# Attention scores in two halves of TensorE's rows, softmax kept in PSUM, one PSUM bank for the input products, and another order of the attention steps

## What is computed

```python
scores = scale * np.matmul(q, k.transpose(0, 1, 3, 2))
keep = is_global | is_local          # first 8 keys, or the 96 keys up to the query
bias = -slopes[:, None, None] * dist[None, :, :]
scores = np.where(keep, scores + bias[None], -1000000000.0)
a = np.exp(scores - np.max(scores, axis=-1, keepdims=True))
a = a / (np.sum(a, axis=-1, keepdims=True) + 1e-09)
x = np.matmul(a, v)                  # then as tokens x 512
h = x @ w_in;  g = np.maximum(h, 0.0) + alpha * np.minimum(h, 0.0);  x = g @ w_out
h = x @ w_in2; g = P(h) / (Q(h) + 1e-06);                            out = g @ w_out2
```

## Time and profile before

| | us |
|---|---|
| Median of 3 runs (647.35 to 648.41) | 648.3 |
| The profiled execution's own time | 649.04 |
| Its span in the profile | 647.2 |
| PE busy | 627.8 |
| DVE, ACT, POOL busy | 460.3, 312.1, 286.8 |

### The profile page before, as it was taken

How to read it: one execution, slowest core, us unless ns; L and a number is a source line. 1 busy time by engine, 2 the same in 40 slices (tenths; PEclk the granted TensorE clock), 3 DMA queues, 4 the chain that set the end, 5 groups by cost and what they waited for, 6 DMA issues and landing times.

```text
span 647.2 us, 9416 instructions
## 1 busy us (share of the span) xinstructions
PE 627.8 (97%) x3048; PEld 503.8 (78%) x3048; DVE 460.3 (71%) x753; ACT 312.1 (48%) x664; POOL 286.8 (44%) x231
## 2 busy tenths in 40 slices
PE   6988999999999999999999999999999999999995
PEld 4666777777877777778888888888888888888884
DVE  6868776665476666646555559988869988599884
ACT  6853333333233333322111167866668766687662
POOL 4777650000000000001444468887757777587772
PEclk9999999999999999999999999999999999999999
DMA  5873321111011111010232210000010000100001
GB/s 161 234 224 102 94 63 37 50 30 30 0 28 42 43 28 39 0 46 20 98 97 99 97 66 0 2 1 1 1 65 0 0 0 0 65 2 0 1 1 69
DMA packets 38933, 31.28 MB, mean 48 GB/s; under 512 B 9008, under 2 KB 33264, under 8 KB 38896
## 3 DMA queue, kind: packets, MB, share of 16 engines
q1 hardware_dynamic: 38896, 30.83, 15.7%
HBM read 27.67 MB, written 3.15 MB: 48 GB/s over the span
## 4 chain that ended last, share of the span: by engine, by line
PE 90%; DVE 3%; issue 2%; DMA 2%; SPq 1%; ACT 1%; POOL 1%; DVEq 0%; POOLq 0%; ACTq 0%
PE ps_h L565 29%; PE ps_y L598 20%; PE ps_y L600 19%; PE ps_o L565 5%; PE ps_s L565 5%; PE ps_s L517 3%; PE ps_o L538 3%; PE ps_o L527 2%; DMA kT<-in_k 2%; PE ps_y L484 1%; SPq L375 1%; DVE g L1010 1%; PE ps_o L508 1%; PE ps_h L496 0%; PE ps_y L482 0%
## 5 line engine op out<-in xcount | busy, mean ns | idle before, releaser
L1227 POOL TENSOR_TENSOR win_lo<-stage,win_hi 128x1024 fp32r<-128x1024 f32 x8 | 19.2, 2405 | 229.9 <-DVE win_hi L1002 229.9
L565 PE MATMUL ps_h<-xy_hi,win_hi 128*128 (+1 forms) x288 | 118.5, 412 | 0.7 <-DVE xy_lo L944 0.7
L565 PE MATMUL ps_h<-xy_lo,win_hi 128*128 (+1 forms) x288 | 112.6, 391 | 0.0
L565 PE MATMUL ps_h<-xy_hi,win_lo 128*128 (+1 forms) x288 | 112.4, 390 | 0.0
L732 ACT ACTIVATE g_hi<-g 128x512 fp32r<-128x512 f32 x48 | 30.3, 631 | 134.7 <-PE ps_y L598 124.1
L1026 DVE RECIPROCAL ps_h<-denom 128x512 f32<-128x512 f32 x24 | 80.6, 3360 | 17.2 <-POOL denom L1234 16.6
L1234 POOL TENSOR_TENSOR denom<-denom,q_abs 128x512 f32<-128x512 f32 x48 | 62.6, 1305 | 62.5 <-ACT denom L752 62.5
L1019 DVE TENSOR_TENSOR g_lo<-g,g_hi 128x512 fp32r<-128x512 f32 x48 | 35.0, 729 | 64.6 <-ACT g_hi L732 64.6
L598 PE MATMUL ps_y<-g_hi,wout_hi 128*128 128x512 f32 x192 | 80.9, 422 | 0.0
L598 PE MATMUL ps_y<-g_hi,wout_lo 128*128 128x512 f32 x192 | 75.2, 392 | 0.0
L600 PE MATMUL ps_y<-wout_hi,g_hi 128*128 128x512 f32 x192 | 74.8, 390 | 0.0
(11 more groups left out here) (139 smaller groups left out, 1258.5 us busy)
## 6 DMA issues: line engine op xcount, KB each, us to landing
stage<-in_w_in SPq DMA_DIRECT2D x8, 512.0 KB, 3.4
stage<-in_w_out SPq DMA_DIRECT2D x8, 512.0 KB, 3.4
qT<-in_q SPq DMA_DIRECT2D x48, 64.0 KB, 2.4
kT<-in_k SPq DMA_DIRECT2D x24, 128.0 KB, 2.4
vv<-in_v SPq DMA_DIRECT2D x24, 128.0 KB, 2.2
out<-xy_raw SPq DMA_DIRECT2D x12, 256.0 KB, 2.2
xy_raw<-in_w_in SPq DMA_DIRECT2D x4, 512.0 KB, 5.0
xy_raw<-in_w_out SPq DMA_DIRECT2D x4, 512.0 KB, 4.1
```

What stands on the lines that cost most here:

```text
L565: mm = pe.matmul(ps_h_at(layer, m), w[:, kc, cut], x[:, blk, kc, :], start=(kc == 0 and n == 0), stop=(kc == KC - 1 and n == 2))
```

## The change

- **Scores.** Each head's score matmul now takes only its own 64 partitions of `qT` and `kT`, so that one uses the upper half of PE's rows and the other the lower, and the two write to different banks, `ps_w[:, 0]` and `ps_w[:, 1]`. The queries come in one transfer and ACT scales them by a factor for each head (a new step "scale"), which the new `qscale` holds.
- **Softmax in PSUM.** DVE adds the distance, multiplies by the slope and takes the extremum in one instruction (`tensor_tensor_reduce`, in place in `ps_w`); ACT takes exponentials in place there; one DVE instruction scales both heads from PSUM into `prob`. `rowmax` and its two instructions go. `ps_w` has one buffer, so a score waits for `prob_ready` of the step before.
- **Banks.** `ps_w` lies over the second bank of `ps_h` and over `ps_s`. While attention runs, all input products use the first bank of `ps_h`, and h(m+2) waits until gate1 of m+1 has been made. In block 2 the banks alternate again.
- **Order.** In the blocks with attention the list is now y(m), split(m+1), h(m+2), g(m+2), instead of h(m+2), g(m+2), y(m), split(m+2). The steps start at place 3 and are 3.2 places apart; turn_prob comes 5 places after the score, and attend(s) stands at the place of score(s+2), right ahead of it. DVE's two turns with attention are written out instead of looped.

```diff
+START, GAP = 3, 3.2
+WITH_SCORE = 6
+LAGS = (-2, "scale"), (0, "score"), (1, "exp"), (2, "norm"), (5, "turn_prob"), (WITH_SCORE, "attend")
...
-            at = int(s * 3.25)
-            for lag, what in ((0, "score"), (1, "exp"), (2, "norm"), (4, "turn_prob"), (5, "attend")):
-                placed.setdefault(at + int(lag), []).append((lag, what, s))
+            for lag, what in LAGS:
+                at = START + int((s + 2) * GAP) if lag == WITH_SCORE else START + int(s * GAP) + lag
+                placed.setdefault(at, []).append((lag, what, s))
...
+            if attention:
+                for m in range(MC):
+                    for half in range(2):
+                        for _, what, s in in_order(4 * m + half):
+                            yield what, s
+                        yield "y", (m, half)
+                    yield "split", m + 1
+                    for half in range(2):
+                        for _, what, s in in_order(4 * m + 2 + half):
+                            yield what, s
+                        yield "h", (m + ahead, half)
+                    yield "g", m + ahead
+                yield "end", None
+                return
...
-                pe.wait_ge(qk_in[pair // 2], (s - pair) * 16 + 48)
-                pe.wait_ge(biased, s * 2)
+                pe.wait_ge(q_scaled, s - STEPS + 1)
+                pe.wait_ge(prob_ready, s * 2)
                 for h in range(2):
-                    mm = pe.matmul(ps_s[:, 2 * P * h:2 * P * (h + 1)], qT[:, pair, h, :],
-                                   kT[:, pair].rearrange("d s t -> d (s t)"), start=True, stop=True)
+                    part = slice(DH * h, DH * h + DH)
+                    mm = pe.matmul(ps_w[:, h, 0:2 * P], qT[part, pair, 1, :], kT[part, pair].rearrange("d s t -> d (s t)"),
+                                   start=True, stop=True)
...
+                    elif layer == 1:
+                        pe.wait_ge(act_ready, MC * BLOCKS)
                     elif not (isinstance(c, int) and c < 2):
-                        pe.wait_ge(act_ready, c - 1)
+                        pe.wait_ge(act_ready, c if alone else c - 1)
...
+                act.activation(qT[:, pair, 1, :], qT[:, pair, 0, :], ACT.Copy, scale=qscale[:, pair:pair + 1]).then_inc(q_scaled, 1)
...
+                    dve.tensor_tensor_reduce(out=ps_w[:, h, 0:2 * P], in0=dist[:, at:at + 2 * P], in1=ps_w[:, h, 0:2 * P],
+                                             scale=slope(2 * pair + h), scalar=LEAST, op0=ALU.add, op1=ALU.min,
+                                             accum_out=negmax[:, i % 2, h:h + 1]).then_inc(biased, 1)
...
+                dve.wait_ge(prob_turned, s - 1)
+                dve.tensor_tensor(prob[:, i % 2], ps_w[:, :, 0:2 * P], rden[:, i % 2, :].unsqueeze(2).to_broadcast([P, 2, 2 * P]),
+                                  ALU.mult).then_inc(prob_ready, 2)
```

More of the change, by code:

```diff
@@ L184, in first_keys, with ps_h_at, bank1 @@
             return 1 if i < PAIRS else 2
-        def ps_h_at(layer, m):
-            return ps_h[:, m % 2, :] if layer == 0 or m % 4 < 2 else (ps_s, ps_o)[m % 2][:, :]
+        def ps_h_at(m):
+            return ps_h[:, m % 2, :] if m % 4 < 2 else (ps_s, ps_o)[m % 2][:, :]
+        def bank1(attention, m):
+            return 0 if attention or m >= MC else (m + 1) % 2
         n_in = sem("n_in")
@@ L371, in load_qk @@
                     sp.wait_ge(scored, s - 2)
-                for h in range(2):
-                    part = slice(DH * h, DH * h + DH)
-                    sp.dma_start(qT[part, two, h, :], q[batch, part, two, tile]).then_inc(qk_in[loaded], 16)
+                if ab:
+                    sp.dma_start(qT[:, two, 0, :], q[batch, :, two, tile]).then_inc(qk_in[loaded], 16)
+                else:
+                    for h in range(2):
+                        part = slice(DH * h, DH * h + DH)
+                        sp.dma_start(qT[part, two, h, :], q[batch, part, two, tile]).then_inc(qk_in[loaded], 16)
                 sp.dma_start(kT[:, two, slot, :], k[batch, :, two, tile]).then_inc(qk_in[loaded], 16)
@@ L540, in attend, with hidden @@
                 mm.then_inc(attended, 1)
-            def hidden(layer, blk, m, half, order, wait_w):
+            def hidden(layer, blk, m, half, order, wait_w, place, alone):
                 c = MC * (blk + BLOCKS * layer) + m
@@ L564, in hidden @@
                     for n, (w, x) in enumerate(parts):
-                        mm = pe.matmul(ps_h_at(layer, m), w[:, kc, cut], x[:, blk, kc, :],
+                        mm = pe.matmul(place, w[:, kc, cut], x[:, blk, kc, :],
                                        start=(kc == 0 and n == 0), stop=(kc == KC - 1 and n == 2))
@@ L609, in run_block @@
                         m, half = arg
[L610 to L614, removed]
+                        nl, nb = (layer, blk) if m < MC else (1, 0) if after == "layer" else (layer, blk + 1)
+                        place = ps_h_at(m) if nl else ps_h[:, bank1(attention, m), :]
+                        hidden(nl, nb, m % MC, half, (order1, order2)[nl], wait_w if m < MC else wait_next, place, attention)
                     elif what == "y":
@@ L629, in _ @@
             for m, half in ((0, 1), (1, 0), (1, 1)):
-                hidden(0, 0, m, half, order1, True)
+                hidden(0, 0, m, half, order1, True, ps_h[:, m, :], False)
             with pe.Fori(0, BLOCKS - 1) as blk:
@@ L957, in score @@
                 for h in range(2):
[L959 to L963, removed]
-                dve.wait_ge(maxed, (s - STEPS) + 1)
-                dve.tensor_scalar(negmax[:, i % 2, :], rowmax[:, i % 2, :], -SCALE, None, ALU.mult).then_inc(negmax_ready, 1)
+                    dve.tensor_tensor_reduce(out=ps_w[:, h, 0:2 * P], in0=dist[:, at:at + 2 * P], in1=ps_w[:, h, 0:2 * P],
+                                             scale=slope(2 * pair + h), scalar=LEAST, op0=ALU.add, op1=ALU.min,
+                                             accum_out=negmax[:, i % 2, h:h + 1]).then_inc(biased, 1)
             def denominator(ab, i):
@@ L1073, in _ @@
             dve.wait_ge(consts_in, 32)
-            for m in range(2):
-                gate1(0, m)
-                split1(0, m)
-            with dve.Fori(0, BLOCKS - 1) as blk:
+            gate1(0, 0, 0)
+            split1(0, 0)
+            gate1(0, 1, 1)
+            for blk in range(BLOCKS - 1):
                 for what, arg in block_events(0, True, "block"):
                     if what == "g":
-                        gate1(blk + arg // MC, arg % MC)
+                        gate1(blk + arg // MC, arg % MC, bank1(True, arg))
                     elif what == "split":
@@ L1256, in _ @@
             filled(pool.memset(ab_sb[:, 8:9], 1.0 + 1e-6))
+            for head in range(HEADS):
+                part = slice(DH * (head % 2), DH * (head % 2) + DH)
+                pool.memset(qscale[part, head // 2:head // 2 + 1], -SCALE / slope(head)).then_inc(scales_ready, 1)
+            pool.wait_ge(scales_ready, HEADS)
             pool.wait_ge(dist_ready, 4)
```

67 lines of the change are left out of this document (35 added, 32 removed).

## The result

| | before | after |
|---|---|---|
| Median (us) | 648.36 (647.35 to 648.61, 4 runs) | 643.25 (641.27 to 645.31, 4 runs) |
| Ratio to before, 95% interval | | 0.993 (0.9905 to 0.9954) |
| Own time of the profiled execution | 649.04 | 645.31 |
| Its span | 647.2 | 643.6 |

A forecast was written before the change was run, and what follows sets the result against it. PE was taken to bound the kernel, busy 627.8 of 647.2 us. Terms -7.4 - 3.0 + 3.0 + 3.3 = -4.1 took the profiled 649.0 to 644.9; the median, 0.7 lower, was forecast at 644.2 us, range 638.0 to 651.5.

The forecast's parts named there:

- Attend and score: PE's attention inserts in two blocks: paired attend and score 1.42 us against 1.67, lone ones included; -7.4 us.
- First transposes: PE's waits before the first transposes of blocks 0 and 1 go, by later place and shorter norm; -3.0 us.
- One buffer for the scores: Score waits for the previous norm, hidden except behind a gate: 0.45 us three times a block; maybe 0.3 at step 3; +3.0.
- One bank for h: h(m+2) waits for gate m+1, but y(m) and inserted attention cover it; no cost.
- Block's end, 0 to 1: y(0) waits for xy_lo because DVE takes end1 behind h(17)'s gate: 2.5 us, then 0.5 more.
- Block's end, 1 to 2: The old order puts h(2) in between, so only 0.3 us of the block-end wait is left.
- Score in row halves: Both heads' score matmuls run side by side on PE: work 0.43 us instead of 0.87, plus changes of shape.
- Rival A: Heads do not run side by side in the score: 14 us more, 658.3 us, slower; chance 0.09.
- rival B: Program order holds inside PE's array, three turns for four in the score: 651.1 us, slower; chance 0.07.
- Rival C: PE's shape changes cost otherwise: 5.6 or up to 11 us less, or some 12 more; chance 0.12 for the low side.
- rival D's second case: DVE and ACT are faster than added up, so the score buffer's 3.0 us goes: 641.2, within the 0.60 range 641 to 647.
- At nothing: ACT's scaling, the single query transfer, POOL's fills and DVE's lighter biasing cost nothing; uncovered scaling at most 0.3 us a step.

The follow-up runs named there:

- e4: Changed kernel with score matmuls over all 128 rows instead of 64 for each head, so the numbers differ; 652.06 us, ratio 1.0075.
- e7: Kernel before with turn_prob and attend 5 and 6 places behind their score instead of 4 and 5; 648.34 us, ratio 1.0002.
- e10: Changed kernel with the transposes 4 places behind their score, as in the kernel before, instead of 5; 659.01 us, ratio 1.0172.
- e6: Changed kernel with attend 7 places behind its own score, taking nine of a block's 14 joint attends away from the score beside them; 654.9 us, ratio 1.0113.
- e9: e6 with the separated attends' ACT and DVE parts queued behind the exponentials of the neighbouring score; 652.56 us, ratio 1.0085.
- e8: e3 with the gate's first DVE instruction made three times in the attention blocks, some 1.6 us more per gate; 653.66 us, ratio 1.009.
- e5: Changed kernel run again unaltered, beside the other runs of its set; 643.41 us, ratio 0.9928.
- e1: Changed kernel with end1 directly behind y(15) for ACT and DVE, ahead of h(17) and its gate; 639.18 us, ratio 0.9874.
- e2: Changed kernel with the norms of steps 1, 6 and 11 one place earlier, ahead of the product's gate on DVE; 642.33 us, ratio 0.9926.
- e3: Changed kernel with both moves, end1 ahead of h(17)'s gate and the norms of steps 1, 6 and 11 ahead of theirs; 637.5 us, ratio 0.9848.

## Why the prediction was right

The total was near, and the terms can be set beside the traces of the kernel before and the changed one, from start to start:

| Term | predicted | measured |
|---|---|---|
| Attend and score | -7.4 | -6.7 |
| First transposes | -3.0 | -3.5 |
| One buffer for the scores | +3.0 | +2.0 |
| One bank for h | 0 | 0 |
| Block's end, 0 to 1 | +3.0 | +3.0 |
| Block's end, 1 to 2 | +0.3 | +0.1 |
| Clock behind the wait | not seen | +1.2 |
| Sum | -4.1 | -3.9 |

The row of attend and score is 40.1 us for the 28 pairs without their waits, 3.4 for the four lone scores and 3.2 for the four lone attends, 46.7 against 53.4. The traces have -4.1 for blocks 0 and 1 and +0.1 for block 2. The total is better than its terms: the score's saving and the clock came out worse by 0.7 and 1.2, the transposes and the one buffer better by 0.5 and 1.0. That these errors cancel is luck, and so is it that the prologue and the tail moved by 1.3 and -1.1 with nothing in the change to explain them.

- **Score in row halves.** Right in kind and nearly in size: side by side, 1.44 us a pair for 1.42, with a change of shape on both sides. The lone score was mis-sized, about 0.84 us for 0.78, so the changes of shape around it cost 0.41 and not 0.35. Rival A is refuted by the record starts and by e4, rival B by the same starts (three turns would span 0.43 us) and by the 1.44 us of a pair. The rule that the Trainium skill states for program order (TensorE: Matmul & The Clock Gate, Part 3) does not describe two matmuls in different halves here: the attend's starts span 0.39 us and the score's about 0.3, where that order would need at least 0.65 (seven turns) and 0.43 (three turns). Rival C did not come either way.
- **First transposes.** The waits went, and they were worth 3.5 us, not 3.0, as a third set of transposes had been late. But the step that named the later place as half of the cause was too simple. e7: the later place without the shorter softmax only moves the wait to attend. e10: the shorter softmax without the later place has no wait for `prob` at the transposes, and yet loses 15.6 us. Place 5 is needed because of ACT's queue and `ps_o`, which the prediction did not look at.
- **One buffer.** Right place, right count, wrong size: 0.33 us for 0.45 each. In the rows above the norm ends 2.52 us behind the gate's start (187.51 to 190.03) where I added up 2.59, and the rest is that PE's own work ahead of the score took about 0.1 longer; the extra 0.3 at step 3 did not come. This is rival D's second case, for about a third of the 3.0. "Hidden elsewhere" holds only for this order of ACT's queue, as e6 and e10 show, and only with attend standing in front of the score, as e9 shows.
- **One bank for h.** Nothing, as said; e8 shows that even 1.6 us more of gate reach it only nine times of 32, six of them by some 0.3 us.
- **Block's end.** Right: from the end of the last turn of h(17) (170.23 + 0.23) to y(0) at 172.86 it is 2.40 us for 2.5, and e5 has 0.57 for 0.5 behind it. The 0.3 between blocks 1 and 2 is too small for the list of waits; block 2 takes 90.0 us, against 89.8 in e1 and 89.9 in the kernel before. What the step left out is the clock behind the wait, 1.2 us in the profiled execution.
- **At nothing.** The scaling, the transfers and the fills show in no wait of PE.

## To carry to other kernels

Before a step is moved by one place, write down for every engine what is then ahead of what in its queue: a copy that waits for PE, put in front of the exponentials, cost by the profiles about 4 of the 11.5 us of e6 and 8 of the 15.6 of e10, though each move looked free on PE. A single buffer for a chain over three engines makes each such shift visible, and neighbours on PE's own stream (attend ahead of score) can be the cover that keeps it hidden. When an engine changes the order at a loop's end, look for the item that has all its inputs and stands behind one that does not; here moving `end1` forward was worth 4 us.

## What was not expected of the hardware

- Two fp32 matmuls of 64 rows each overlap on PE just as two of 64 columns do: four records of 256 columns start within some 0.3 us instead of 0.65. Entering and leaving the halved array costs some 0.36 us around a lone attend and 0.41 around a lone score (0.80 and 0.84 less the work of 0.44 and 0.43), and going from column halves directly to row halves saves 0.21 (1.44 against 0.84 + 0.81).
- Behind an idle time of 2.2 us of PE, the granted clock fell to its lower level for 3 to 4 us in five of seven profiled executions (the changed kernel, e2, e4, e6 and e10; not in e5 and e9), which cost 1.2 to 1.4 us from y(0) to the next h. In the five without that idle time (before, e1, e3, e7, e8) it did not fall there, nor behind the idle time of 2.02 us at 58.87 in the kernel before. The same program did both (the changed kernel and e5), so what decides it is open.
